# A fused attention and two-layer kernel: the next batch's transposes two head slots later, the exponents' sums added in pairs, the half chunks' gate products in two banks and their output sums two to a bank

## What is computed

```python
q_d = q.reshape(B, H, Sd, factor, D).mean(axis=3)      # the same for k and v; Sd = 144
out_up = np.repeat(sm_attn(q_d, k_d, v_d), factor, axis=2)
mask = np.abs(pos[:, None] - pos[None, :]) < factor
scores = np.where(mask, scale * np.matmul(q, k.transpose(0, 1, 3, 2)), -1000000000.0)
out_local = np.matmul(softmax(scores), v)
x = (out_up + out_local)              # then as 2304 tokens x 512
xn = x / np.sqrt(np.mean(x * x, axis=-1, keepdims=True) + 1e-06) * rms_g
g = xn @ w_gate                       # 512 x 1536
y = (g * (1.0 / (1.0 + np.exp(-g))) * (xn @ w_val)) @ w_out
out = (s * np.maximum(y @ w_in, 0.0) ** 2 + b) @ w_out2     # 512 x 2048, 2048 x 512
```

## Times and profile before

| | |
|---|---|
| median of 3 executions | 1042.65 us (1041.69 to 1043.13) |
| the profiled execution | 1041.87 us, of which 1039.8 us from the first to the last instruction (the span) |
| busy PE, DVE, ACT, POOL | 966.9, 537.4, 332.0, 412.8 us |
| mean granted TensorE clock | 0.93 of full speed |

### The profile page before, as it was taken

One profiled execution on the slowest core, in us unless ns is written; L12 is line 12 of the kernel. 1 busy time (PEld: TensorE's weight loads), 2 busy tenths in 40 slices (PEclk: granted clock), 3 DMA queues, 4 the chain that ended last, 5 costly groups with the idle time before them and its releaser, 6 DMA issues.

```text
span 1039.8 us, 13258 instructions
## 1 busy us (share of the span) xinstructions
PE 966.9 (93%) x5080; PEld 783.5 (75%) x5080; DVE 537.4 (52%) x791; ACT 332.0 (32%) x722; POOL 412.8 (40%) x209
## 2 busy tenths in 40 slices
PE   2788887896999999999999999999999999999997
PEld 1566677795777767777777798887888888888896
DVE  5579856676676676556453233334443443443343
ACT  2433654322432332242224244323222222222232
POOL 5888829886578487545650055200000000000000
PEclk9555579998999999999999999999999999999999
DMA  9973346421133132101202144101100200000010
GB/s 314 295 217 122 103 126 196 123 91 61 48 106 101 40 95 91 56 18 31 71 13 84 79 126 137 43 1 41 41 1 1 81 1 0 29 33 1 1 41 21
DMA packets 55502, 80.00 MB, mean 77 GB/s; under 512 B 10960, under 2 KB 38064, under 8 KB 54032
## 3 DMA queue, kind: packets, MB, share of 16 engines
q1 hardware_dynamic: 53424, 74.45, 23.6%
q10 hardware_dynamic: 2016, 4.72, 1.2%
HBM read 67.35 MB, written 11.80 MB: 76 GB/s over the span
## 4 chain that ended last, share of the span: by engine, by line
PE 75%; POOL 7%; DVE 7%; issue 3%; DMA 3%; ACT 2%; SPq 2%; DVEq 0%; ACTq 0%; POOLq 0%
PE bank L698 23%; PE bank L806 6%; PE bank L808 6%; PE bank L824 6%; PE bank L807 6%; PE bank L825 6%; PE bank L826 6%; PE bank L721 4%; PE bank L719 4%; PE bank L720 4%; POOL prod L522 3%; POOL prod L508 3%; DVE sc L528 1%; DVE csum L1241 1%; DMA vs<-in_v_dram 1%
## 5 line engine op out<-in xcount | busy, mean ns | idle before, releaser
L508 POOL TENSOR_TENSOR prod<-qs,ks 128x896 f32<-128x896 f32 x80 | 175.2, 2211 | 97.8 <-DVE sc L528 87.6
L522 POOL TENSOR_TENSOR prod<-sc,vs 128x896 f32<-128x896 f32 x80 | 151.1, 1997 | 62.1 <-DVE x L538 39.8
L845 DVE SCALAR_TENSOR_TENSOR r<-bank,r 128x512 f32<-128x512 f32 (+1 forms) x80 | 51.1, 638 | 183.8 <-ACT r L833 183.8
L808 PE MATMUL bank<-y_h,w2i_l 128*128 128x512 f32 (+1 forms) x320 | 117.7, 368 | 0.0
L698 PE MATMUL bank<-x_h,wg_h 128*128 128x256 f32 (+1 forms) x288 | 93.1, 348 | 19.5 <-ACT u L728 17.7
L719 PE MATMUL bank<-h_h,wo_h 128*128 128x256 f32 (+1 forms) x288 | 107.4, 373 | 3.8 <-issue 3.8
L740 DVE TENSOR_TENSOR bank<-bank,u 128x256 f32<-128x256 f32 (+1 forms) x72 | 40.5, 562 | 134.1 <-PE bank L698 120.9
L698 PE MATMUL bank<-x_h,wv_h 128*128 128x256 f32 (+1 forms) x288 | 104.3, 377 | 0.0
L833 ACT ACTIVATE r<-bank 128x512 f32<-128x512 f32 (+1 forms) x80 | 44.4, 555 | 183.8 <-PE bank L808 183.1
L721 PE MATMUL bank<-h_h,wo_l 128*128 128x256 f32 (+1 forms) x288 | 97.9, 340 | 0.0
L720 PE MATMUL bank<-h_l,wo_h 128*128 128x256 f32 (+1 forms) x288 | 97.2, 338 | 0.0
(11 more groups left out here) (123 smaller groups left out, 1963.5 us busy)
## 6 DMA issues: line engine op xcount, KB each, us to landing
raww<-in_moe_w_out_dram SPq DMA_DIRECT2D x14, 512.0 KB, 3.8
rawk<-in_k_dram SPq DMA_DIRECT2D x4, 1152.0 KB, 8.3
rawq<-in_q_dram SPq DMA_DIRECT2D x4, 1152.0 KB, 11.1
rawv<-in_v_dram SPq DMA_DIRECT2D x4, 1152.0 KB, 8.7
ks<-in_k_dram SPq DMA_DIRECT2D x16, 280.0 KB
vs<-in_v_dram SPq DMA_DIRECT2D x16, 280.0 KB, 3.6
raww<-in_moe_w_in_dram SPq DMA_DIRECT2D x8, 512.0 KB, 3.5
y_raw<-y_scr SPq DMA_DIRECT2D x4, 1024.0 KB, 4.8
```

The lines of the kernel that those rows point to most:

```text
L508: pool.tensor_tensor(dst, qv, kv, ALU.mult).then_inc(prod_ready, 1)
L522: pool.tensor_tensor(dst, pv, vv, ALU.mult).then_inc(prod_ready, 1)
L808: last = pe.matmul(o, w2i_l[:, m, kk, :], y_h[t % 2][:, kk, 0:w], start=False, stop=kk == DT - 1)
```

## The change

The edits, in the order of the diff:

- Pieces of the next batch's pooled q and k are transposed from slot 5 of a batch on, not from slot 3 (UNIT_FROM). `pool_q` and `pool_v` of the next batch move two slots later with them.
- The reductions of tile 0 are spread otherwise: the last q-k reduction in slot 14 and not 13, the p-v reductions in slots 17 to 28 and not 16 to 25. The softmax, the adding of the pooled result, the squares and the inverse root move by one or two slots; `normalise` of x's first half stands in slot 31 and not 30.
- csum gets a second column that holds 1e-9. `finish_pooled` adds the two columns with one reduction into rsum and inverts it, where before a `tensor_scalar` added 1e-9 and multiplied by 4. The factor goes into the copy of the transposed exponents (scale 1/4).
- In chunks 0 and 1 `gate` writes bank 0 in even steps and bank 6 in odd steps, and u has two halves. `gate(s)` waits for the silu of step s - 2, `silu(s)` for the multiplication of step s - 2. The four output sums of these chunks lie two to a bank in YB[0] and YB[1], and `store_y` copies a bank at once (2 instructions, not 4).
- On DVE three reductions of tile 1 stand ahead of chunk 0: after the head loop come the low part of piece 3, reductions 0 and 1, then `split_lo`, then reduction 2. The table QK1_AT ends in step 8 (before: 10), and PV1_AT starts in step 10 of chunk 0 (before: step 0 of chunk 1). The softmax of tile 1 is taken in steps 8 and 9, its squares in steps 3 and 6 of chunk 1 ahead of `hidden_hi`, and `normalise` is split around `hidden_hi` in step 7.
- On PE the transposes of x for chunk 0 stand ahead of the p-v matmuls of heads 30 and 31.
- On SP: q of batch 1 is loaded ahead of k of batch 1, the three small loads stand later, and so do the stores of the pooled v; two q-k windows and two v windows of tile 1, and the store of batch 2's result, move ahead.

```diff
-UNIT_FROM = 3
-PV0_AT = {16: (0, 1), 17: (2, 3), 18: (4,), 19: (5, 6), 20: (7,), 21: (8, 9), 22: (10,), 23: (11, 12), 24: (13, 14), 25: (15,)}
+UNIT_FROM = 5
...
+PV0_AT = {17: (0,), 18: (1, 2), 19: (3,), 20: (4,), 21: (5, 6), 22: (7,), 23: (8, 9), 24: (10,), 25: (11,), 26: (12, 13), 27: (14,), 28: (15,)}
...
-QK1_AT = {0: (0, 1), 1: (2, 3), 2: (4,), 3: (5, 6), 4: (7,), 5: (8,), 6: (9,), 7: (10, 11), 8: (12,), 9: (13, 14), 10: (15,)}
+QK1_AT = {0: (3,), 1: (4, 5), 2: (6, 7), 3: (8,), 4: (9, 10), 5: (11,), 6: (12,), 7: (13, 14), 8: (15,)}
...
-        csum = place(at, "csum", [P, 2, 2 * H], F32)
+        csum = place(at, "csum", [P, 2, 2 * H, 2], F32)
+        rsum = place(at, "rsum", [P, 2, H], F32)
...
+        def gate_bank(s):
...
+        def u_part(s):
...
+            c, m = divmod(s, M1)
+            w = CHUNKS[c][2]
+            return slice(s % 2 * w, s % 2 * w + w) if w < W_ else slice(0, w)
...
+        def sums_of(c, dt):
...
+            w = CHUNKS[c][2]
+            return YB[dt // 2][:, dt % 2 * w:dt % 2 * w + w] if c < 2 else YB[dt][:, 0:w]
...
-            wait(pe, u_ready, s)
-            first_in(pe, GB, wg_h, wg_l, s, m == 0).then_inc(gate_done, 1)
+            w = CHUNKS[c][2]
+            wait(pe, u_ready, s - 1 if 0 < s < 2 * M1 else s)
+            if s == 1:
+                pe.wait_ge(co_ready, 2 * B - 1)
+            first_in(pe, gate_bank(s), wg_h, wg_l, s, m == 0).then_inc(gate_done, 1)
...
-                o = YB[dt][:, 0:w]
+                o = sums_of(c, dt)
...
-                pe.matmul(o, wo_h[:, m, cols], h_h[:, s % 3, 0:w], start=m == 0, stop=False)
+                pe.matmul(o, wo_h[:, m, cols], h_h[:, s % 3, 0:w], start=m == 0 and not (c < 2 and dt % 2), stop=False)
...
-                last = pe.matmul(o, wo_l[:, m, cols], h_h[:, s % 3, 0:w], start=False, stop=m == M1 - 1)
+                last = pe.matmul(o, wo_l[:, m, cols], h_h[:, s % 3, 0:w], start=False, stop=m == M1 - 1 and not (c < 2 and dt % 2 == 0))
...
-            w = CHUNKS[s // M1][2]
+            c, m = divmod(s, M1)
+            w = CHUNKS[c][2]
...
-            wait(act, hf_ready, s)
-            act.activation(u[:, 0:w], GB[:, 0:w], ACT.Silu).then_inc(u_ready, 1)
+            wait(act, hf_ready, s - 1 if w < W_ and m else s)
+            act.activation(u[:, u_part(s)], gate_bank(s)[:, 0:w], ACT.Silu).then_inc(u_ready, 1)
...
-            for dt in range(DT // 2 if c == NCH - 2 else DT):
-                act.activation(y_st[t % 2][:, dt, col0:col0 + w], YB[dt][:, 0:w], ACT.Copy).then_inc(y_evac, 1)
+            if c < 2:
+                for n in range(DT // 2):
+                    act.activation(y_st[t % 2][:, 2 * n:2 * n + 2, col0:col0 + w], YB[n][:, :].rearrange("p (d c) -> p d c", d=2), ACT.Copy).then_inc(y_evac, 2)
+            else:
+                for dt in range(DT // 2 if c == NCH - 2 else DT):
+                    act.activation(y_st[t % 2][:, dt, col0:col0 + w], YB[dt][:, 0:w], ACT.Copy).then_inc(y_evac, 1)
...
-            store_vd(2)
...
+            load_v(sp, 0, 3)
...
-            load_v(sp, 0, 3)
+            store_vd(2)
...
+            load_qk(sp, 1, 0)
+            load_qk(sp, 1, 1)
...
-            store_vd(3)
...
+            load_v(sp, 0, 6)
+            store_vd(3)
+            load_v(sp, 0, 7)
...
-            load_v(sp, 0, 6)
-            load_v(sp, 0, 7)
-            load_qk(sp, 1, 0)
-            load_qk(sp, 1, 1)
+            load_v(sp, 1, 0)
+            load_v(sp, 1, 1)
+            store_co(2)
...
-            store_co(2)
...
-            load_v(sp, 1, 0)
+            pool.memset(csum[:, :, :, 1:2], 1e-9)
...
-                    act.activation(cpT[0:JH, g % 2, :], CPT[g % 2][0:JH, 0:2 * J], ACT.Copy).then_inc(cpt_evac, 1)
+                    act.activation(cpT[0:JH, g % 2, :], CPT[g % 2][0:JH, 0:2 * J], ACT.Copy, scale=1.0 / FAC).then_inc(cpt_evac, 1)
+                if n == 15:
+                    softmax_exp(act, 0)
...
-                                       accum_out=csum[0:JH, b % 2, 2 * h + a:2 * h + a + 1]).then_inc(cexp, 1)
+                                       accum_out=csum[0:JH, b % 2, 2 * h + a, 0:1]).then_inc(cexp, 1)
...
-                if n == 14:
-                    softmax_exp(act, 0)
-                if n == 23:
+                if n == 24:
...
-                if n == 24:
+                if n == 25:
...
-                if n == 25:
+                if n == 26:
...
-                if n == 27:
+                if n == 28:
+                    weight_hi(act, 3)
+                if n == 29:
...
-                if n == 28:
+                if n == 30:
...
-                if n == 30:
+                if n == 31:
...
-                if n == 31:
-                    weight_hi(act, 3)
...
+                if c == 0 and m == 9:
+                    softmax_exp(act, 1)
+                if c == 1 and m == 3:
+                    squares(act, 1, 0)
+                if c == 1 and m == 6:
+                    squares(act, 1, 1)
+                if c == 1 and m == 7:
+                    normalise(act, (0, 1), 2)
...
-                if c == 0 and m == 11:
-                    softmax_exp(act, 1)
-                if c == 1 and m == 4:
-                    squares(act, 1, 0)
-                if c == 1 and m == 6:
-                    squares(act, 1, 1)
...
-                    normalise(act, range(FAC), 2)
+                    normalise(act, (2, 3), 2)
...
-                cb = csum[0:JH, b % 2, 8 * g:8 * g + 8]
-                c_link(dve.tensor_scalar(cb, cb, 1e-9, float(FAC), ALU.add, ALU.mult))
-                c_link(dve.reciprocal(cb, cb))
+                rs = rsum[0:JH, g, :]
+                c_link(dve.tensor_reduce(rs, csum[0:JH, b % 2, H * g:H * (g + 1), :], op=ALU.add, axis=AX.X))
+                c_link(dve.reciprocal(rs, rs))
...
-                                  over(csum[0:JH, b % 2, 8 * g:], [[1, 2], [2, 4], [0, D]]), ALU.mult).then_inc(co_ready, 1)
+                                  over(rsum[0:JH, g, 0:], [[1, 2], [2, 4], [0, D]]), ALU.mult).then_inc(co_ready, 1)
...
-                if b < B - 1 and h < 2:
-                    pool_q(b + 1, h)
...
-                    pool_v(b + 1, h - 2)
+                    pool_q(b + 1, h - 2)
...
+                if b < B - 1 and 4 <= h < 6:
+                    pool_v(b + 1, h - 4)
...
-                if n == 13:
+                if n == 14:
...
-                if n == 14:
+                if n == 15:
...
-                if n == 26:
+                if n == 28:
...
-                if n == 27:
+                if n == 29:
...
-                if n == 29:
+                if n == 30:
...
+            weight_lo(dve, 3)
+            qk_reduce(dve, 1, 0)
+            qk_reduce(dve, 1, 1)
...
-            weight_lo(dve, 3)
+            qk_reduce(dve, 1, 2)
...
-                    if m == 10:
+                    if m == 8:
...
-                    if m == 11:
+                    if m == 9:
+                        softmax_norm(dve, 1)
...
-                        softmax_norm(dve, 1)
+                for n in PV1_AT.get((c, m), ()):
+                    pv_reduce(dve, 1, n)
...
-                    for n in PV1_AT.get(m, ()):
-                        pv_reduce(dve, 1, n)
-                    if m == 4:
+                    if m == 2:
...
+                    if m == 5:
+                        add_pooled(dve, 1, 1)
...
-                        add_pooled(dve, 1, 1)
-                    if m == 7:
...
+                if n == HEADS + 1:
+                    pe.wait_ge(ctr_evac, UNITS * B)
+                    transpose_x(pe, 0, 0)
+                    transpose_x(pe, 0, 1)
...
-                if n == HEADS + 1:
-                    transpose_x(pe, 0, 0)
-                    transpose_x(pe, 0, 1)
...
-                if s == LAG:
+                if s == LAG + 2 * M1:
```

26 lines of the change are left out of this document (13 added, 13 removed).

## The result

The changed kernel took 1028.02 us (median of four executions, 1026.82 to 1028.86), the kernel before 1042.72 beside it: a ratio of 0.986, 95% interval 0.9842 to 0.9877. That is 14.7 us faster where 26.8 were forecast. The direction was right, the size was about half, and the range ended at 1028.0, just short of the median.

A forecast was written before the change was run, and what follows sets the result against it. PE's matmuls bound chunk 2 onward; before it, POOL's tile 1 products set its start. Gains of 9.6 (first gate), 5.6 (POOL's restart), 9.6 (POOL's idle time) and 2.0 (behind the last product) took 1042.65 to 1015.9 us; range 1004 to 1028.

## What to carry to other kernels

When an edit makes an engine wait, follow that wait through every queue behind it until it either ends in idle time that costs nothing or comes back to the engine that was waited for: here POOL, DVE and ACT, 84, 68 and 33% busy, held one another up. In a program with a hand-written order, ask for a product as late as the consumer allows and write what others wait for ahead of your own wait, if its input is there; the same edit cost 0.4% where the load came late. And a cause is not shown by a right sum: it took undoing edits alone, and doing them alone, to tell the sums, slots, loads and tables apart.
